# Attention scores in two phases over row halves, a new order of the value product, and weight pieces spread over 14 heads

## What is computed

```python
B, H, S, D = 4, 8, 576, 64
scores = q @ k.T / sqrt(D);  scores = where(pos_i // 64 >= pos_j // 64, scores, -1e9)
attn = exp(scores - max(scores));  attn = attn / (sum(attn) + 1e-9)
x = heads_side_by_side(attn @ v)                 # B x 576 x 512
h = relu(x @ w_in);  u, v = h[..., :512], h[..., 512:]
v_n = (v - mean(v)) / sqrt(var(v) + 1e-6)
y = (u * (w_spatial @ v_n + b_spatial)) @ w_out
out = y + relu(layernorm(y) * g_ln @ w_ch1) @ w_ch2
```

## Time and profile before

| | before |
|---|---|
| median of 3 runs | 902.29 us (899.33 to 902.93) |
| the profiled execution | 902.78 us, of which 900.2 us from the first to the last instruction |
| PE busy | 866.7 us, 96% of the span |
| PE weight loads | 705.6 us, 78% |
| DVE, ACT, POOL busy | 363.3, 284.5 and 200.9 us (40%, 32%, 22%) |
| chain that ended last, by engine | PE 89%, issue 4%, DVE 2%, POOL 2% |
| mean granted clock of TensorE | 0.987 |

### The profile page before, as it was taken

How to read it: one execution, slowest core, us unless ns; L and a number is a source line. 1 busy time by engine, 2 the same in 40 slices (tenths; PEclk the granted TensorE clock), 3 DMA queues, 4 the chain that set the end, 5 groups by cost and what they waited for, 6 DMA issues and landing times.

```text
span 900.2 us, 13334 instructions
## 1 busy us (share of the span) xinstructions
PE 866.7 (96%) x5000; PEld 705.6 (78%) x5000; DVE 363.3 (40%) x806; ACT 284.5 (32%) x752; POOL 200.9 (22%) x289
## 2 busy tenths in 40 slices
PE   7779999999999999999889999999999999999998
PEld 3445677766777668776788999989999999998997
DVE  5556664436644366433765422132132122122111
ACT  5455553345543454433434311111111111111110
POOL 3666342532424224340353100000000000000000
PEclk9889999999999999999999999999999999999999
DMA  6442121122221222102524201101100200200100
GB/s 200 156 133 69 65 67 50 57 74 72 67 67 41 82 64 67 40 2 77 195 85 147 82 1 39 68 1 38 67 0 35 70 0 35 70 0 35 36 1 36
DMA packets 37680, 56.02 MB, mean 62 GB/s; under 512 B 2749, under 2 KB 20157, under 8 KB 37630
## 3 DMA queue, kind: packets, MB, share of 16 engines
q1 hardware_dynamic: 37630, 55.34, 18.8%
HBM read 45.90 MB, written 9.44 MB: 61 GB/s over the span
## 4 chain that ended last, share of the span: by engine, by line
PE 89%; issue 4%; DVE 2%; POOL 2%; DMA 1%; ACT 1%; SPq 0%; ACTq 0%; POOLq 0%; DVEq 0%
PE psum L959 22%; PE psum L961 22%; PE psum L960 22%; PE psum L922 7%; PE psum L936 6%; PE psum L951 3%; PE psum L954 3%; PE psum L917 2%; PE psum L1033 1%; DVE row_sum L719 1%; ACT probs L525 1%; PE psum L925 0%; POOL rstd L452 0%; DMA qk_raw<-qk 0%; POOL unit_raw L491 0%
## 5 line engine op out<-in xcount | busy, mean ns | idle before, releaser
L881 DVE SCALAR_TENSOR_TENSOR h_r<-psum,h_r 128x384 fp32r<-128x384 f32 x96 | 53.5, 557 | 287.2 <-ACT h_r L673 287.2
L673 ACT ACTIVATE h_r<-psum 128x384 fp32r<-128x384 f32 x96 | 47.2, 491 | 340.6 <-PE psum L961 340.6
L959 PE MATMUL psum<-xn_r,units_r 128*128 128x384 f32 x384 | 129.7, 338 | 0.0
L961 PE MATMUL psum<-xn_r,units_r 128*128 128x384 f32 x384 | 129.4, 337 | 0.0
L960 PE MATMUL psum<-xn_r,units_r 128*128 128x384 f32 x384 | 128.9, 336 | 0.0
L711 DVE TENSOR_REDUCE neg_max<-psum 128x1 f32<-128x128 f32 (+4 forms) x160 | 83.7, 540 | 79.3 <-PE psum L925 53.2
L961 PE MATMUL psum<-units_r,h_r 128*128 128x512 f32 x288 | 113.8, 395 | 0.0
L960 PE MATMUL psum<-units_r,h_r 128*128 128x512 f32 x288 | 113.6, 394 | 0.0
L525 ACT ACTIVATE probs<-psum,neg_max 128x128 f32<-128x128 f32 (+4 forms) x160 | 90.1, 566 | 73.0 <-DVE neg_max L711 72.1
L959 PE MATMUL psum<-units_r,h_r 128*128 128x512 f32 x288 | 112.0, 389 | 0.0
L441 POOL TENSOR_SCALAR probs<-probs,row_inv 128x128 f32<-128x128 f32 (+4 forms) x160 | 89.9, 578 | 95.7 <-DVE row_inv L724 95.7
(11 more groups left out here) (95 smaller groups left out, 1485.0 us busy)
## 6 DMA issues: line engine op xcount, KB each, us to landing
qk_raw<-qk SPq DMA_DIRECT2D x32, 576.0 KB, 3.8
unit_raw<-w_ch SPq DMA_DIRECT2D x32, 256.0 KB, 3.1
y_norm<-y_scratch SPq DMA_DIRECT2D x6, 768.0 KB, 5.6
y_res<-y_scratch SPq DMA_DIRECT2D x6, 768.0 KB, 4.6
out<-y_res SPq DMA_DIRECT2D x18, 256.0 KB, 2.1
v_raw<-vN SPq DMA_DIRECT2D x16, 256.0 KB, 2.8
y_scratch<-mix_buf SPq DMA_DIRECT2D x16, 256.0 KB, 2.0
w_raw<-w_in SPq DMA_DIRECT2D x8, 256.0 KB, 4.4
```

Source lines behind the costliest of these rows:

```text
L673: act.activation(h_hi[:, f % HR, :], h_bank[:, f % 2, 0:CHUNK], ACT.Relu).then_inc(h_hi_done, 1)
L881: dve.scalar_tensor_tensor(h_lo[:, f % HR, :], h_bank[:, f % 2, 0:CHUNK], 0.0, h_hi[:, f % HR, :].bitcast(F32), ALU.max, ALU.subtract).the ...
L959: pe.matmul(dst, a_hi, b_hi, start=start, stop=False)
L961: return pe.matmul(dst, a_lo, b_hi, start=False, stop=stop)
```

## The change

- The scores of a head are computed in two phases. `score_first` computes tile 3 on the low row half and tiles 2 and 0 on the high one, 512 keys each; `score_second` computes tile 4 on both (288 keys each) and then tile 1 on both (128 keys each). The tiles of a head are handled in the order 3, 0, 2, 1, 4 everywhere (`TILES`), and `scored` counts four to a head. The maxima of a phase wait for all its scores. The exponentials of tiles 0 and 2 wait for both of their maxima, and so do those of tiles 1 and 4 (`PEAKS`).
- The scores have banks 0 and 1 for the first phase and 2 and 3 for the second while there are no mixer groups, and later banks 1 and 2 for the second, which then waits for the first phase's exponentials. The banks of transposes and mixer groups change places.
- On PE, step 0 is now attend(n-1) and then the first phase of head n+1, step 1 the transposes of tile 3, step 2 those of tiles 0 and 2, step 3 the second phase of head n+1 and the transposes of tile 1, step 4 those of tile 4. DVE and ACT copy the value product's result in step 0 and do the first phase's softmax in step 1 and the second's in step 3.
- The matmuls of the value product are issued left 0, right 0, right 1, left 1, right 2, right 3, left 2, right 4, left 3, and `pv_done` counts two to a head.
- One weight piece is split in each of the heads 0 to 10 and two in each of the heads 11 to 13. The first four are loaded ahead of the loop, the others four pieces ahead. Each kind of mixer group waits for its own pieces only. The second qk load stands ahead of the first v load, and g_cols is loaded behind the first four pieces.

```diff
--- before.py
+++ after.py
@@ -149,13 +149,12 @@
         psum = ctx.enter_context(nc.psum_tensor("psum", [P, 8, 512], F32))
-        s_bank = psum[:, 0:3, :]
-        t_bank = psum[:, 3:5, :]
+        m_bank = psum[:, 3:5, :]
         o_bank = psum[:, 5, :]
-        m_bank = psum[:, 6:8, :]
+        t_bank = psum[:, 6:8, :]
         acc_bank = psum[:, 0:3, :]
-        h_bank = psum[:, 3:5, :]
-        xt_bank = psum[:, 5:8, :]
+        h_bank = psum[:, 6:8, :]
...
@@ -230,19 +229,35 @@
...
-        DVE_TILES, ACT_TILES = [0, 1, 3], [2, 4]
+        DVE_TILES, ACT_TILES = [3, 0, 1], [2, 4]
...
+            m, u = (n, TILES[AT[t] - 2]) if AT[t] >= 2 else (n - 1, TILES[AT[t] - 2 + NT])
...
-        def invert_at(t):
-            return 2 if t >= 3 else 1
+        TILES = [3, 0, 2, 1, 4]
+        PEAKS = {3: 1, 0: 3, 2: 3, 1: 5, 4: 5}
+        AT = [TILES.index(t) for t in range(NT)]
+        FIRST = 3
+
+        def second_banks(n):
+            return psum[:, 2:4, :] if n < H else psum[:, 1:3, :]
+
+        def score_of(n, t):
+            if t == 0:
+                return psum[:, 1, KEYS[2]:KEYS[2] + KEYS[0]]
+            if t == 2:
+                return psum[:, 1, 0:KEYS[2]]
+            if t == 3:
+                return psum[:, 0, 0:KEYS[3]]
+            if t == 1:
+                return second_banks(n)[:, :, HALF:HALF + P]
+            return second_banks(n)[0:LAST, :, 0:HALF]
...
@@ -266,6 +281,8 @@
...
             if b == 0 and g < 2:
+                if g == 0:
+                    eng.wait_ge(exped, NT * H)
                 return
...
@@ -297,10 +314,13 @@
...
-        PER_SLOT_W = -(-len(pieces) // H)
+        PIECES_PER_HEAD = [1] * H + [1, 1, 1, 2, 2, 2]
+        PIECES_V, PIECES_S = 2 * KD, 2 * KD + NT
...
         def pieces_at(n):
-            return range(PER_SLOT_W * n, min(PER_SLOT_W * (n + 1), len(pieces))) if n < H else []
+            at = sum(PIECES_PER_HEAD[:n])
+            return range(at, at + PIECES_PER_HEAD[n]) if n < len(PIECES_PER_HEAD) else []
...
@@ -330,14 +350,14 @@
...
-                    sp.wait_ge(scored, NT * (n - QS + 1))
+                    sp.wait_ge(scored, 4 * (n - QS + 1))
...
@@ -366,17 +386,20 @@
...
             load_qk(0)
+            load_qk(1)
             load_v(0)
-            load_qk(1)
+            load_qk(2)
+            for i in range(WR):
+                load_piece(i)
             sp.dma_start(g_cols[:, :], gT).then_inc(misc_loaded, 16)
-            load_qk(2)
             for n in range(HEADS):
                 if n + 3 < HEADS:
                     load_qk(n + 3)
                 if n % 2 == 0 and n // 2 + 1 < HEADS // 2:
                     load_v(n // 2 + 1)
                 for i in pieces_at(n):
-                    load_piece(i)
+                    if i + WR < len(pieces):
+                        load_piece(i + WR)
...
@@ -471,15 +494,15 @@
...
                     if step == 0:
-                        for t in range(3):
+                        for t in TILES[:FIRST]:
                             normalise(n, t)
                     elif step == 1:
-                        for t in range(3, NT):
+                        for t in TILES[FIRST:]:
                             normalise(n, t)
                         if n + 2 < HEADS:
                             scale_q(n + 2)
-                    if 2 <= step and step - 2 < len(pieces_at(n)):
-                        split_piece(pieces_at(n)[step - 2])
+                    if 3 <= step and step - 3 < len(pieces_at(n)):
+                        split_piece(pieces_at(n)[step - 3])
...
@@ -513,24 +536,23 @@
...
-                act.wait_ge(maxed, NT * n + t + 1)
+                act.wait_ge(maxed, NT * n + PEAKS[t])
...
-                if t == NT - 1:
+                if t in TILES[FIRST:]:
                     dst = dst.rearrange("p (a n) -> p a n", a=2)
...
@@ -600,34 +620,32 @@
...
                     if step == 0:
-                        if n + 1 < HEADS:
-                            for t in range(3):
-                                exp_tile(n + 1, t)
-                    elif step == 1:
                         if n >= 1:
                             output_right(n - 1)
-                        piece(n, 1)
+                    elif step == 1:
+                        if n + 1 < HEADS:
+                            for t in TILES[:FIRST]:
+                                exp_tile(n + 1, t)
                         if n and n % H == 0:
                             for k in range(KD):
                                 split_x(n // H - 1, k)
                     elif step == 2:
                         copy_transposed(n, 2)
-                        if n + 1 < HEADS:
-                            exp_tile(n + 1, 3)
                     elif step == 3:
                         if n + 1 < HEADS:
-                            exp_tile(n + 1, 4)
+                            for t in TILES[FIRST:]:
+                                exp_tile(n + 1, t)
                     else:
                         copy_transposed(n, 4)
-                    if step == 0:
+                    if step == 2:
                         piece(n, 0)
                     if step == 4:
-                        piece(n, 2)
...
@@ -703,19 +721,18 @@
...
-                r, k, s = ROWS[t], KEYS[t], n % 2
-                dve.wait_ge(scored, NT * n + t + 1)
...
+                r, s = ROWS[t], n % 2
+                dve.wait_ge(scored, 4 * n + (2 if t in TILES[:FIRST] else 4))
...
@@ -785,37 +802,35 @@
...
                     if step == 0:
-                        if n + 1 < HEADS:
-                            for t in range(3):
-                                max_tile(n + 1, t)
-                    elif step == 1:
                         if n >= 1:
                             output_left(n - 1)
-                        copy_transposed(n, 0)
-                        copy_transposed(n, 1)
+                    elif step == 1:
+                        if n + 1 < HEADS:
+                            for t in TILES[:FIRST]:
+                                max_tile(n + 1, t)
+                        copy_transposed(n, 3)
                         if n and n % H == 0:
                             for k in range(KD):
                                 split_x(n // H - 1, k)
                     elif step == 2:
+                        copy_transposed(n, 0)
                         if n + 1 < HEADS:
-                            max_tile(n + 1, 3)
                             invert(n + 1, 0)
                     elif step == 3:
                         if n + 1 < HEADS:
-                            max_tile(n + 1, 4)
-                        copy_transposed(n, 3)
+                            for t in TILES[FIRST:]:
+                                max_tile(n + 1, t)
+                        copy_transposed(n, 1)
                     else:
                         if n + 1 < HEADS:
                             invert(n + 1, 1)
@@ -902,38 +917,53 @@
...
-            def score_tile(n, t):
-
-                s, r = n % QS, ROWS[t]
-                if t == 0:
-                    pe.wait_ge(q_scaled, n + 1)
-
-                free = NT * n + [-1, 0, 0, 1, 3][t]
-                if free > 0:
-                    pe.wait_ge(exped, free)
-                if t == NT - 1:
-                    for half in range(2):
-                        g = slice(BLOCK * half, BLOCK * (half + 1))
-                        last = pe.matmul(s_bank[0:r, 1 + half, 0:HALF], qk_raw[g, s, 0, P * t:P * t + r],
-                                         qk_raw[g, s, 1, HALF * half:HALF * (half + 1)], start=True, stop=True)
+            def score(n, dst, half, rows, keys):
+
+                return pe.matmul(dst, qk_raw[half, n % QS, 0, rows], qk_raw[half, n % QS, 1, keys],
+                                 start=True, stop=True)
+
+            def mask(dst, half):
+                return pe.matmul(dst, row_pick[half, :], row_mask[half, :], start=False, stop=True,
+                                 skip_group_check=True)
+
+            LOW, HIGH = slice(0, BLOCK), slice(BLOCK, P)
+
+            def rows_of(t):
+                return slice(P * t, P * t + ROWS[t])
+
+            def score_first(n):
+
+                pe.wait_ge(q_scaled, n + 1)
+                if n >= 1:
+                    pe.wait_ge(exped, NT * n)
+                score(n, score_of(n, 3), LOW, rows_of(3), slice(0, KEYS[3]))
+                score(n, score_of(n, 2), HIGH, rows_of(2), slice(0, KEYS[2]))
+                mask(score_of(n, 2)[:, KEYS[2] - BLOCK:KEYS[2]], HIGH)
+                score(n, score_of(n, 0), HIGH, rows_of(0), slice(0, KEYS[0]))
+                mask(score_of(n, 0)[:, KEYS[0] - BLOCK:KEYS[0]], HIGH).then_inc(scored, 1)
+                mask(score_of(n, 3)[:, KEYS[3] - BLOCK:KEYS[3]], LOW).then_inc(scored, 1)
+
+            def score_second(n):
+
+                if n >= H:
+                    pe.wait_ge(exped, NT * n + FIRST)
+                for half, part in enumerate((LOW, HIGH)):
```

(63 more changed lines are left out.)

68 lines of the change are left out of this document (32 added, 36 removed).

## The result

The changed kernel takes 947.12 us (median of 4 runs, 946.72 to 952.49) against 902.61 us before (4 runs, 899.33 to 903.5): a ratio of 1.051, 95% interval 1.047 to 1.056. The forecast was 916.5 us with a range to 928. The sign was right, the size was off by 31 us.

A forecast was written before the change was run, and what follows sets the result against it. TensorE's own sequence was taken to bound the rounds. The profiled 902.8 us, +14.5 for three rounds, -0.2 for the last value product and 0 for the first heads gave 917.1, less 0.5: 916.5 us, range 894 to 928.

The forecast's parts named there:

- TensorE's own sequence: In the rounds of eight heads: TensorE is busy 109.96 of 110.73 us, so every wait put into it is paid.
- Work removed: TensorE per mixer head: scores fall from 2.92 to 2.11 us, value product from 1.73 to 1.55; net gain 0.06.
- The rival of passes in program order: Value product: the new column order brings nothing or costs up to 0.37 us x 32, total 928; chance 0.03.
- Waits added: TensorE per round: waits for softmax, copies and the split of x add 8.4 us; old waits of 1.75 go.
- the split of x: Head that starts a batch: ACT's split queues behind three exponentials, so the first mixer group waits 1.3 us.
- The early frame: First eight heads, one value product to the next: a latency chain of 9.5 us, against a mean of 9.96.
- A round: Eight mixer heads: -0.5 - 1.8 - 1.75 + 8.4 = +4.3 us, to about 115; three rounds +14.5.
- The main case: Whole kernel: about +14 us, within 907 to 925 us; chance 0.50.
- a rival at 0.15: Clock drops at new gaps: 1.7 us lost per early frame, 2 in every second round, total 928; chance 0.15.
- Net 0: First eight heads: 89.7 us against 91.20, with 1.5 given back for clock drops; bounds -8 and +12.

The follow-up runs named there:

- the filled one: The changed kernel with idle matmuls of the identity added in TensorE's gaps, order and waits untouched: 926.7 us, ratio 1.028.
- a kernel that is 1.4% faster: The kernel before with only the spread weight pieces and the new column order of the value product: 888.54 us, ratio 0.986.

## Why the prediction was right or wrong, point by point

- **TensorE's own sequence is the time in the rounds, and every wait is paid.** Right. With the clock held, a round of 117.15 us is its forecast work and waits to within 2.1 us.
- **Work removed.** First phase 1.21 us forecast; in the round it is 235.91 to 237.12, 1.21. Value product 1.55 forecast, 1.51 measured. The rival of passes in program order is out, as the new order shortened it. The Trainium skill (TensorE: Matmul & The Clock Gate, Part 3, what overlaps and what doesn't) has matmuls start and end strictly in program order. The prediction's estimate from that rule was about 1.9 us for the new product, and the measured 1.51 decides against it. The second phase was mis-sized: 0.90 forecast, 1.09 measured, 1.5 us a round. Tile 4 takes the 0.64 us forecast (228.94 to 229.58), tile 1 with its mask 0.45 (to 230.03) for 0.26. The Trainium skill (TensorEngine Tiling (Array Packing), Key Properties) says that a change of tiling mode drains TensorE. The phase has one such change more than tile 4 alone had, behind tile 1, but no run here prices it by itself.
- **Waits added.** Right in mechanism and size: 1.25 us from tile 4's transposes to the product in a covered head; in the fourth head 3.39 for 3.46; in the second 1.64 of idle, 0.91 over the common 0.73, for 0.95; for tile 2's transposes 1.48 us of idle and for the split of x 1.30, where 1.7 and 1.3 were forecast. The early frame was 9.5 us forecast and is 9.60 where no drop lengthens it: three of seven in the changed kernel, six of seven in the filled one.
- **A round.** 115 us was the sum. With the clock held it is 117.15, and 1.5 of the 2.1 missing are the second phase. Of the 31 us that the forecast lacked, the 10 that filling does not bring back are 6.7 in the three rounds (4.4 of them second phases), 2.1 up to the end of the first heads, and 1.1 behind the last head.
- **The clock: the step that failed.** The main case put the clock at nothing in the rounds and at 1.5 us in the first heads. It stood as a rival at 0.15, at 928 us, with one round in two losing 2 us, because one gap of 2.59 us had passed at full clock. In the changed kernel each of the last two rounds has four drops of 3.4 us, behind gaps of 1.64 to 2.70 us and behind the pair of 1.48 and 1.30 at the split of x. In the first eight heads four of the seven frames are lengthened by drops, 17 us at half clock in all. Filling the gaps recovers 20 us of the 31 that the forecast lacked. One quiet gap was weak evidence: the old early heads, at a clock of 0.85, had shown what repeated gaps do, and the main case should have carried it. The rival's own terms (10.5 us in the first heads and 2 in half of three rounds) add up to 930, not 928.
- **First eight heads.** "Net 0" hid two large terms. The old 9.96 us mean, which held the waits for pieces and the old drops, was compared with a new 9.5. Shown separately, the spread is worth some 19 us in this stage, and the longer path (7.20 to about 9.6) takes 17 of them. The clock then took 6.6 us, for the 1.5 allowed. The first product came 0.6 us later, where 1.7 was forecast.
- **What was not seen.** The prediction does not mention that the first phase waits for all exponentials of the head before. In the changed kernel the product in front of it waits longer, so it costs nothing there; it is what spoils the version with the product moved back.
- **Small slips.** 917.1 less 0.5 is 916.6, and POOL is busy 38.75 us of the 110.73, not 41. Neither bears on the result.

A kernel in which the exponential of tile 1 starts before the maximum of tile 4 is taken, which would shorten the longest chain by about 0.45 us (an estimate, the length of that exponential), was not tried: the two tiles share banks, and ACT would read one while DVE reads it.

What stays open is which gaps bring a drop. In the changed kernel gaps of 1.63 and 2.51 us brought one in the second and third rounds and none in the first, and in the kernel with only the long gaps filled the same unfilled pair at the split of x had a drop in one round and none in the next.

## What to carry to other kernels

When a matmul stream waits for a copy of its own last output, put other work of the stream between the two before shortening anything else: waits of 0.94 us a head, and what followed from them, cost 27 to 32 us here, more than was saved inside the matmuls. A gap in a dense stream has two prices, its length and the clock behind it; where a change adds repeated gaps like those here (1.3 to 2.7 us), count both, and fill them with idle matmuls to tell the two apart. Price each part of a bundled change alone: here one part was worth -10 us, one -3, the two phases cost 32 (12 with the gaps filled) and the move 27 on top of them, and the bundle as a whole hid a kernel that is 1.4% faster.

## What the runs showed of the hardware

- Gaps of 1.64 us were followed by 3.4 us at half clock in the second and third rounds of the changed kernel, while one of 2.59 us in the kernel before was not the earlier trace rows. With the product moved alone, six gaps of 1.50 and 1.69 us in the rounds brought one drop. The length of a gap alone does not tell.
- With two to eight idle fp32 matmuls of 128 columns in each gap the granted clock was 1.00 from 26.5 to 494 us; ahead of that, from 12.5 us on, it was at half, and eight of them took 3.7 us.
- A value product split over two column halves ran in 1.51 us in the new order of its matmuls and in 1.73 in the old one; its streaming is estimated at 1.33 us, from 800 columns to a half, two passes, and 0.43 us for a pass of 512.
